# Pooled v with its keys on the partitions: by DMA through a scratch in HBM, or by copies and transposes

## The chip, the cores and the metric

The program runs on one core of a Trainium2 chip. The metric is the device time of one execution in microseconds, the median of several runs. TensorE (PE), VectorE (DVE), ScalarE (ACT), GpSimd (POOL) and SyncE (SP) each run their own instruction list in order and wait for each other on semaphores. SP computes nothing here: it issues nearly all DMAs, which all go into one queue that 16 DMA engines serve.

## What is computed

Three layers in a row, all in fp32:

```python
# attention, B=8 batches, H=8 heads, S=576 queries, D=64; keys and values pooled by 8 -> SP=72
k_p = k.reshape(B, H, Sp, 8, D).mean(axis=3);  v_p = v.reshape(B, H, Sp, 8, D).mean(axis=3)
attn = softmax(q @ k_p.T / sqrt(D))
x = (attn @ v_p)                       # as [4608, 512]
# soft mixture of experts: 32 slots, 8 experts, w1 [8,512,1024], w2 [8,1024,512]
logits = x @ phi
d = softmax(logits, over tokens);  slot_input = d.T @ x
slot_out[e] = relu(slot_input[e] @ w1[e]) @ w2[e]
x = softmax(logits, over slots) @ slot_out
# last layer: h = x @ w_in, h * softmax(h), layer norm, @ w_out
```

The kernel never builds `x`. For the logits it multiplies attn with (v_p @ phi). For the slot inputs it forms `dat = d.T @ attn` for each batch (32 slots by 72 keys of each head) and then `dat @ v_p`. The second product contracts over the 72 keys, so it needs v_p with its keys on the partitions: the tile `v72` [72, 8 heads, 64].

## The kernel before

**Stage 1, attention (about 0 to 178 us).** Loop over 8 batches `b`, each with 5 tiles of queries. The instruction lists of PE, ACT and DVE are written by hand as `step(b, par, t, ...)` with t = 1 to 5, software-pipelined: step t does the scores of tile t+2, the transposed q of tile t+3, the transposed attn of tile t and the logits of tile t-1. `par` is the parity of the batch and picks one of two buffers. Batch 0 is unrolled, batches 1 to 6 run in a loop of two batches a turn, and the last batch has a tail of its own.

**Loads.** For each batch SP loads v (two DMAs, `load_v`, lines 403 and 406), q (four `qb` DMAs of 1024 pieces of 256 bytes, line 427, and two `ql`, line 430), from batch 3 on also one 2 MB half of an expert's weights (`load_w`, lines 436 and 438), and k (two DMAs). The loop of SP is at lines 468 to 479: it waits until v of batch b is pooled (`v_pooled`), loads v and q of batch b+1 and a weight half, waits until k of batch b+1 is pooled and loads k of batch b+2. `load_v(7)` is in its iteration b=6. After it come the weight halves whose place in SBUF comes free late: n=5, n=7, n=6, then the output weights `wo_raw` (`load_out`, line 449: chunks 0 to 3, 4, 5 and 6, 7), parts of halves 8 (`wnine`) and 9 (`wten`), and, in stage 2, halves 10 to 15.

**Pooling.** `fold` (lines 380 to 394) adds the 8 neighbours in three levels; level 2 writes `kp` or `vp` and signals `k_pooled` or `v_pooled`. Most of it is done by POOL, between the normalisations of attn (`norm`, line 577).

**The way of v.** `vT_t` transposes `vp` on PE into the bank `b_head` (line 1419); `vT_evac` on ACT copies it into `vpad` (v transposed, with its pooled keys in the free dimension, 6 copies); `wphi_t` and `vphi_t` make v_p @ phi of it. For `v72`, the heads' columns are copied out of `vpad` into `vT`: `vT_close` on ACT for batches 0 and 1, `vT_copy` on DVE for the others (two copies of 64x288). Then `v72_t(b)` at step 2 transposes them back on PE (4 transposes, line 1459, behind three waits), and `v72_evac(b)` at step 3 copies the bank to `v72` on ACT. `slot_t(b)` reads `v72` at step 5 of the next batch (line 1553) and signals `slot_ps`.

**The tail of the last batch.** After step 1 of batch 7 PE goes through scores, logits and `dat_t` of batch 6, `lmax_t`, `slot_t(6)`, then waits for `wo_in0` (chunks 0 to 4 of `wo_raw`), runs `mb_t`, `col_sum(0)`, waits for `wo_in1` (chunks 5 to 7), runs `col_sum(1)` (line 1640, 8 matmuls each), `dat_t(7)`, `datT_t(7)` and `slot_t(7)`. The order is fixed, so everything after waits with it.

**Stage 2, experts (178 to 222 us):** `hid_t(e)` (line 1698) and `so_t(e)` (line 1720) for the 8 experts, each waiting for its half of the weights. **Stage 3 (from 222 us):** the last layer, 36 output tiles of 128 tokens, PE busy nearly throughout.

Of the kernel before, what the change touches and what calls it, by code (L numbers as in the profile page):

```python
# [29 lines left out]
F32 = mybir.dt.float32  # L30
# [5 lines left out]
P = 128  # L36
# [45 lines left out]
def build(nc, q, k, v, phi, w1, w2, w_in, w_out, g_ln, out):  # L82
    with ExitStack() as ctx:
# [40 lines left out]
        vp = bump("vp", [P, EVEN, D])  # L124
# [15 lines left out]
        vT = bump("vT", [P, PAIRS, SP])  # L140
        vT_end = place[0]
# [32 lines left out]
        assert attn_end + HALF // MC <= vpad_end and attn_end + 2 * HALF // MC <= vT_end  # L174
# [205 lines left out]
        def fold(engine, name, raw, pooled, b, level):  # L380
# [19 lines left out]
        def _(sp):  # L400
# [49 lines left out]

            load_first_k()
# [9 lines left out]
            sp.wait_ge(sem("v_pooled"), 1)  # L461
            load_v(1)
# [24 lines left out]
            load_w(3, 0)  # L487
            sp.wait_ge(sem("qT_ps"), B * TILES - 1)
# [3 lines left out]
            sp.wait_ge(sem("vT_closed"), B)  # L492
# [5 lines left out]
            sp.wait_ge(sem("v72_ps"), B)  # L498
# [55 lines left out]
        def _(pool):  # L554
# [14 lines left out]
            def v_fold(b, level):  # L569
                fold(pool, "v", vraw, vp, b, level)  # L570
# [9 lines left out]
            v_fold(0, 0)  # L580
# [5 lines left out]
            v_fold(1, 0)  # L586
            norm((0, 0, 3))

            def step(b, par, t, k_next, v_next):
                norm(ahead(b, par, t + 1))  # L590
                if t == 1 and v_next:
                    v_fold(b + 1, 1)
                    v_fold(b + 1, 2)
# [5 lines left out]
                if t == 5 and k_next:  # L599
                    v_fold(b + 2, 0)  # L600
# [82 lines left out]
        def _(act):  # L683
# [25 lines left out]
            def vT_close(b):  # L709

                act.wait_ge(sem("vT_sb"), b + 1)
                for hh in range(2):
                    c = 1 + hh * HEAD
                    last = copy(vT[hh * D:(hh + 1) * D, :, :], vpad[hh * D:(hh + 1) * D, :, c:c + SP])
                last.then_inc(sem("vT_closed"), 1)

# [30 lines left out]

            def v72_evac(b, par):
                act.wait_ge(sem("v72_ps"), b + 1)
# [1150 lines left out]
```

## Time and profile before

| | us |
|---|---|
| median of 3 runs (lowest, highest) | 452.81 (450.83, 453.76) |
| the profiled execution, first to last instruction | 449.2 |
| of it attention | about 178 |
| of it experts | about 44 |
| of it last layer | about 227 |

The granted TensorE clock is 1.00 of full speed in every stretch. PE is busy 96% of the span, VectorE 71%, ScalarE 60%, GpSimd 56%. The 16 DMA engines are busy for nearly the whole first 212 us. Durations of single instructions are pipelined: the busy time of a group of matmuls overlaps that of the next, so what a group adds to the time is read from the chain of work that ended last, where pieces don't overlap.

### The profile page before, as it was taken

What the parts mean: (1) busy time and instruction counts of PE and PEld (TensorE: products, weight loads), DVE (VectorE), ACT (ScalarE), POOL (GpSimd) and SP (SyncE); (2) the same over time, 40 slices, a digit from 0 to 9 for tenths busy, and PEclk for the clock granted to TensorE, in tenths of its full rate; (3) what the DMA queues carried; (4) which work ended last, traced back from release to release, by engine and by line L of the source; (5) the groups of instructions that cost most, each with busy time, mean ns of one, the idle gap of its engine ahead of it and who ended that gap; (6) DMA issues with size and microseconds to landing.
All of it is one profiled execution on the core that took longest, in us unless ns stands there. A gap on an engine that the chain in (4) does not pass through costs nothing.

```text
span 449.2 us, 10103 instructions
## 1 busy us (share of the span) xinstructions
PE 431.4 (96%) x3492; PEld 335.0 (75%) x3492; DVE 316.9 (71%) x558; ACT 267.4 (60%) x604; POOL 251.0 (56%) x347
## 2 busy tenths in 40 slices
PE   6899999999999998999899999999999999999997
PEld 6676787778778775445578788888888888888886
DVE  5888697877879665736598987777777777777311
ACT  2588878778787854134387665655565555666310
POOL 2569977878887230112034336766766667666540
PEclk9999999999999999999999999999999999999999
DMA  8969959898999998999500276676666766666642
GB/s 258 296 190 239 257 151 267 329 283 279 341 211 359 388 393 285 392 389 396 207 1 24 48 163 118 132 144 137 134 136 140 141 134 134 132 118 136 154 81 47
DMA packets 125951, 91.71 MB, mean 204 GB/s; under 512 B 105176, under 2 KB 105440, under 8 KB 124000
## 3 DMA queue, kind: packets, MB, share of 16 engines
q1 hardware_dynamic: 120752, 82.08, 66.8%
q10 hardware_dynamic: 5168, 9.24, 6.0%
q8 instruction: 17, 0.28, 0.3%
q14 instruction: 14, 0.11, 0.1%
HBM read 66.13 MB, written 9.44 MB: 168 GB/s over the span
## 4 chain that ended last, share of the span: by engine, by line
PE 75%; DVE 7%; ACT 6%; DMA 6%; issue 3%; POOL 1%; SPq 1%; DVEq 0%; ACTq 0%
PE banks L1835 13%; PE banks L1837 13%; PE banks L1836 13%; PE banks L1412 5%; DMA wslot<-in_moe_w 5%; PE banks L1475 3%; PE banks L1393 3%; PE banks L1807 3%; ACT vpad L685 2%; PE banks L1499 2%; PE banks L1535 2%; PE banks L1698 2%; PE banks L1506 2%; PE banks L1720 2%; DVE attn L1039 1%
## 5 line engine op out<-in xcount | busy, mean ns | idle before, releaser
L1835 PE MATMUL banks<-wo_hi,uh 128*128 128x512 f32 x280 | 109.6, 391 | 0.1
L1837 PE MATMUL banks<-wo_hi,ul 128*128 128x512 f32 x280 | 109.0, 389 | 0.0
L1836 PE MATMUL banks<-wo_lo,uh 128*128 128x512 f32 x280 | 108.9, 389 | 0.0
L653 POOL TENSOR_TENSOR ul<-u_col,uh 128x1024 fp32r<-128x1024 f32 x30 | 72.2, 2407 | 16.2 <-ACT uh L685 15.0
L577 POOL TENSOR_TENSOR attn<-attn,srec 128x576 f32<-128x576 f32 (+1 forms) x40 | 43.2, 1082 | 39.6 <-DVE srec L1051 39.4
L950 ACT ACTIVATE sq<-u,st 128x1024 f32<-128x1024 f32 x36 | 41.5, 1153 | 39.9 <-DVE u L1284 39.9
L1835 PEld LDWEIGHTS banks<-wo_hi,uh 128*128 128x128 f32 x280 | 52.6, 188 | 11.4 <-DVE ul L1301 0.5
L1837 PEld LDWEIGHTS banks<-wo_hi,ul 128*128 128x128 f32 x280 | 52.5, 188 | 11.0
L1836 PEld LDWEIGHTS banks<-wo_lo,uh 128*128 128x128 f32 x280 | 52.6, 188 | 10.7
L1284 DVE SCALAR_TENSOR_TENSOR u<-banks,ex 128x1024 f32<-128x1024 f32 x35 | 42.7, 1223 | 22.3 <-ACT ex L941 22.2
L1274 DVE TENSOR_REDUCE st<-banks 128x1 f32<-128x1024 f32 x35 | 42.6, 1218 | 17.5 <-PE banks L1807 17.5
L941 ACT ACTIVATE ex<-banks,st 128x1024 f32<-128x1024 f32 x35 | 39.0, 1114 | 17.1 <-DVE st L1274 16.7
L685 ACT ACTIVATE uh<-u_col 128x1024 fp32r<-128x1024 f32 x30 | 31.8, 1060 | 28.4 <-DMA u_col<-u_blk 14.5
L1315 DVE TENSOR_SCALAR osb<-banks,rs 128x512 f32<-128x512 f32 x35 | 26.0, 742 | 19.2 <-PE banks L1837 19.2
L1412 PE MATMUL banks<-kblk,qT 128*128 128x144 f32 x256 | 37.8, 291 | 1.0 <-DVE attn L1039 0.9
L1294 DVE STREAM_TRANSPOSE u_blk<-u 128x1024 f32<-128x1024 f32 x30 | 37.4, 1246 | 1.9
L1412 PEld LDWEIGHTS banks<-kblk,qT 128*128 128x128 f32 x256 | 33.1, 190 | 3.7 <-issue 3.5
L639 POOL TENSOR_SCALAR st<-st 128x1 f32<-128x1 f32 x36 | 6.9, 190 | 51.6 <-ACT sq L950 51.3
L1033 DVE TENSOR_REDUCE smax<-banks 128x8 f32<-128x576 f32 (+1 forms) x40 | 27.4, 685 | 10.9 <-PE banks L1412 10.5
L728 ACT ACTIVATE attn<-attn 128x576 f32<-128x576 f32 (+1 forms) x40 | 25.5, 636 | 14.8 <-DVE attn L1039 14.4
L1046 DVE TENSOR_REDUCE ssum<-attn 128x8 f32<-128x584 f32 (+1 forms) x40 | 27.8, 694 | 4.9 <-ACT attn L728 4.6
L685 ACT ACTIVATE aT<-banks 128x512 f32<-128x512 f32 (+1 forms) x80 | 28.7, 403 | 2.1 <-PE banks L1475 1.0
(197 smaller groups left out, 792.8 us busy)
## 6 DMA issues: line engine op xcount, KB each, us to landing
wslot<-in_moe_w SPq DMA_DIRECT2D x13, 2048.0 KB, 13.6
u_col<-u_blk SPq DMA_DIRECT2D x240, 64.0 KB, 2.2
qb<-in_q SPq DMA_DIRECT2D x32, 256.0 KB, 6.3
out<-osb ACTq DMA_DIRECT2D x32, 256.0 KB, 2.5
vraw<-in_v SPq DMA_DIRECT2D x8, 640.0 KB, 5.4
kraw<-in_k SPq DMA_DIRECT2D x7, 640.0 KB, 5.9
vraw<-in_v SPq DMA_DIRECT2D x8, 512.0 KB, 4.0
kraw<-in_k SPq DMA_DIRECT2D x7, 512.0 KB, 5.0
```

Of the source, the lines that this page charges most:

```text
L577: pool.tensor_tensor(a, a, per_head(srec[bit(tile)], t)[:, :, :, None].to_broadcast([P, tile_pairs(t), 2, SP]), ALU.mult) \
L653: pool.tensor_tensor(ul[par][:, :, :].rearrange("p c (q t) -> p (c q) t", q=4), v, uh[par][:, :, :].bitcast(F32).rearrange("p c (q t) -> p ...
L685: return act.activation(o, i, ACT.Copy, scale=scale)
L941: act.activation(ex[par][:, :, :], h_banks(par), ACT.Exp, bias=st[k % STATS]["nmax"][:, :], accum_out=st[k % STATS]["den"][:, :]).then_inc ...
L950: act.activation(sq[par][:, :], u[k % URING][:, :], ACT.Square, scale=-float(FF), bias=st[k % STATS]["usum"][:, :], accum_out=st[k % STATS ...
L1274: dve.tensor_reduce(st[k % STATS]["nmax"][:, :], h_banks(k % 2), AX.XY, ALU.max, negate=True).then_inc(sem("nmax"), 1)
L1284: dve.scalar_tensor_tensor(u[k % URING][:, :].rearrange("p (a n) -> p a n", a=2), h_banks(par), 1.0, ex[par][:, :, :], ALU.mult, ALU.mult, ...
L1294: dve.transpose(u_blk[slot][:, :, :, k % 2, :].rearrange("p c q t -> p (c q) t"), u[k % URING][:, :].rearrange("p (b f) -> p b f", f=BLK)) \
L1412: last = pe.matmul(s_view[:, j, 0:2 * SP], qT[bit(tile)][:, j, :], kblk[par][:, j, :], start=True, stop=True)
L1835: pe.matmul(ps[4 + par], uh[par][:, c, :], wo_hi[:, c, :], start=(c == 0), stop=False)
L1836: pe.matmul(ps[4 + par], uh[par][:, c, :], wo_lo[:, c, :], start=False, stop=False)
L1837: last = pe.matmul(ps[4 + par], ul[par][:, c, :], wo_hi[:, c, :], start=False, stop=(c == FC - 1))
```

## The change

`v72` no longer goes through `vT` and PE. As soon as `vp` is pooled, SP writes it to a scratch `pooled_v` in HBM (`spill_v`, two DMAs), and reads it back with the keys on the partitions (`load_v72`, five DMAs of 16 or 8 partitions). `vp` has two buffers. `vT`, `vT_close`, `vT_copy`, `v72_t` and `v72_evac` are gone. The division by 8 that `vT` carried moves to the accumulated denominator, at the end of the stage.

```diff
@@ tiles and the fold
-        vp = bump("vp", [P, EVEN, D])
+        vp = [bump("vp0", [P, EVEN, D])]
-        vT = bump("vT", [P, PAIRS, SP])
+        vp.append(bump("vp1", [P, EVEN, D]))
+                if name == "v" and not (isinstance(b, int) and b < 2):
+                    engine.wait_ge(sem("pooled_v_out"), (b - 1) * 32)
@@ SP
+            def spill_v(b):
+                for a, n in enumerate((EVEN, ODD)):
+                    sp.dma_start(row(pooled_v, b % 2)[0:n, :, a, :].rearrange("n i d -> i n d"), vp[b % 2][a::2, 0:n, :]).then_inc(sem("pooled_v_out"), 16)
+            def load_v72(b):
+                if b >= 2:
+                    sp.wait_ge(sem("slot_ps"), b - 1)
+                sp.wait_ge(sem("pooled_v_out"), 32 * (b + 1))
+                for n in range(EVEN):
+                    i = row(pooled_v, b % 2)[n].rearrange("(h g) a d -> (g a) h d", h=H)
+                    if n < ODD:
+                        c = 4 * POOL * (n % 2) + 2 * POOL * (n // 2)
+                        o = v72[b % 2][c:c + 2 * POOL, :, :]
+                    else:
+                        o, i = v72[b % 2][8 * POOL:SP, :, :], i[0::2]
+                    sp.dma_start(o, i).then_inc(sem(f"v72_in{b % 2}"), 16)
             sp.wait_ge(sem("v_pooled"), 1)
+            spill_v(0)
             load_v(1)
             load_q(1, 1, (1, 2, 3, 4))
             sp.wait_ge(sem("k_pooled"), 2)
             load_k(2)
+            load_v72(0)
             for b in range(1, 7):
                 sp.wait_ge(sem("v_pooled"), b + 1)
+                spill_v(b)
                 load_v(b + 1)
...
                     load_k(b + 2)
+                load_v72(b)
             load_w(2, 1)
+            sp.wait_ge(sem("v_pooled"), B)
+            spill_v(B - 1)
...
             load_w(3, 0)
+            load_v72(B - 1)
             sp.wait_ge(sem("qT_ps"), B * TILES - 1)
             load_out(0, WO_EARLY - 1, 0)
...
-            sp.wait_ge(sem("vT_closed"), B)
             load_part(8, 0, 1)
...
-            sp.wait_ge(sem("v72_ps"), B)
             load_part(8, 1, 2)
@@ ACT: v72_evac (step 3), vT_close (batches 0 and 1) removed
@@ DVE: vT_copy (step 4) removed
-            dve.tensor_scalar(accd1[:, :], acc_den[:, :], TINY, None, ALU.add)
+            dve.tensor_scalar(accd1[:, :], acc_den[:, :], TINY, float(POOL), ALU.add, ALU.mult)
@@ PE
-            def vT_t(b, early=False):
+            def vT_t(b, par):
                 pe.wait_ge(sem("v_pooled"), b + 1)
-                if early:
-                    pe.wait_ge(sem("kT_sb"), b + 1)
-                else:
-                    pe.wait_ge(sem("v72_sb"), b)
-                rows_T("vT", vp)
+                pe.wait_ge(sem("kT_sb"), b + 1)
+                rows_T("vT", vp[par])
-                if t == 2:
-                    v72_t(b)
@@ slot_t
-                pe.wait_ge(sem("v72_sb"), b + 1)
+                pe.wait_ge(sem(f"v72_in{par}"), (b - par) * 40 + 80)
@@ tail
-            v72_t(B - 1)
...
-            pe.wait_ge(sem("v72_sb"), B)
+            pe.wait_ge(sem("vphi_sb"), B)
```

In `pooled_v` (2, 5, 64, 2, 64) the row of 64 floats is the innermost dimension, and neighbouring rows belong to the two values of `a`, so each piece of a spill and of a load is 256 bytes: 576 pieces (147 KB) each way and batch.

## Rows read from the trace of the kernel before

**Rows 1.** Page, 40 slices of the span: busy tenths of PE and of the DMA engines
```profile
PE   6899999999999998999899999999999999999997
DMA  8969959898999998999500276676666766666642
```
**Rows 2.** Window of one batch: PE, PEld, DVE, ACT, POOL busy, clock, DMA, GB/s
```profile
84.70:104.15 19.45, 19.31 (x238) 15.16 (x238) 15.82 (x37) 15.50 (x49) 15.73 (x12) 1.00 0.98 290
```
**Rows 3.** Chain that ended last, in order of time (start, us): v72_t(1) and v72_t(6)
```profile
46.99 0.44 PE banks L1459 x4
...
145.25 0.44 PE banks L1459 x4
145.69 0.44 PE banks L1393 x4
```
**Rows 4.** Timeline (start, us): v72_t(7) and what follows; one batch's copies
```profile
164.32 0.61 PE L1459 MATMUL banks<-ident,vT 128*72 128x128 f32 x4
165.08 0.63 PE L1499 MATMUL banks<-aT,vphi 128*32 128x128 f32 x10 [0.15 <-ACT aT L685]
...
88.92 0.58 ACT L685 ACTIVATE v<-banks 72x512 f32<-72x512 f32 x1
...
95.12 0.96 DVE L1065 COPY vT<-vpad 64x288 f32<-64x288 f32 x2
```
**Rows 5.** Timeline of SP, iteration b=4 and the start of the next
```profile
85.41 0.47 SPq L403 DMA_DIRECT2D vraw<-in_v  x1
...
96.17 0.77 SPq L406 DMA_DIRECT2D kraw<-in_k  x1
104.85 0.47 SPq L403 DMA_DIRECT2D vraw<-in_v  x1
```
**Rows 6.** DMA packets: only q pieces, 111 to 114 us; then queue 1, 300 to 400 us
```profile
DMA packets 2608, 0.66 MB, mean 220 GB/s; under 512 B 2608, under 2 KB 2608, under 8 KB 2608
...
q1 hardware_dynamic: 36761, 8.86, 53.5%
```
**Rows 7.** GB/s in 40 slices of 1 us, from 112 us; then from 150 us
```profile
GB/s 217 219 215 259 410 397 406 414 455 430 420 51 0 57 147 391 389 304 273 217 218 218 196 142 328 336 383 354 371 414 422 426 414 403 393 389 383 385 387 387
...
GB/s 387 387 393 385 383 385 399 410 401 414 410 410 379 389 399 412 373 375 207 393 402 387 352 356 373 80 270 256 121 215 383 266 404 410 426 414 414 414 401 418
```
**Rows 8.** DMAs issued 75 to 77 us: KB, us to landing; and when POOL reads the k
```profile
kraw<-in_k SPq DMA_DIRECT2D x1, 640.0 KB, 10.7
...
88.29 2.92 POOL L386 TENSOR_TENSOR kraw<-kraw 128x1280 f32<-128x1280 f32 x1
```
**Rows 9.** Chain, in order of time: slot_t(4) and slot_t(5)
```profile
136.31 0.36 PE banks L1553 x16
...
155.74 0.36 PE banks L1553 x16
```
**Rows 10.** Timeline of SP, from v(7) to the last chunks of wo
```profile
124.69 0.47 SPq L403 DMA_DIRECT2D vraw<-in_v  x1
...
134.54 9.61 SPq L438 DMA_DIRECT2D wslot<-in_moe_w  x2
...
154.78 0.37 SPq L449 DMA_DIRECT2D wo_raw<-in_moe_w_out  x1
...
165.02 0.33 SPq L446 DMA_DIRECT2D wnine<-in_moe_w  x1
167.10 0.89 SPq L449 DMA_DIRECT2D wo_raw<-in_moe_w_out  x2
```
**Rows 11.** DMAs issued 167.4 to 169.2 us: KB, us to landing (the last chunk of wo)
```profile
wo_raw<-in_moe_w_out SPq DMA_DIRECT2D x1, 256.0 KB, 4.8
```
**Rows 12.** Timeline of PE: col_sum, dat_t(7) (PEld: weight loads of the second half)
```profile
172.48 1.92 PE L1640 MATMUL banks<-wo_raw,gT 128*32 128x512 f32 x16
...
173.37 0.13 PEld L1640 LDWEIGHTS banks<-wo_raw,gT 128*32 128x32 f32 x4 [0.30 <-issue]
...
216.20 1.92 PE L1720 MATMUL banks<-wslot,hz 128*32 128x512 f32 x16 [1.01 <-DMA wslot<-in_moe_w]
```

More of the change, by code:

```diff
@@ L79, with build @@
 FC = FF // P
-def build(nc, q, k, v, phi, w1, w2, w_in, w_out, g_ln, out):
+def build(nc, q, k, v, phi, w1, w2, w_in, w_out, g_ln, pooled_v, out):
     with ExitStack() as ctx:
@@ L139, in build @@
         vphi = [bump("vphi0", [P, NB, SLOTS])]
-        vT = bump("vT", [P, PAIRS, SP])
-        vT_end = place[0]
+        vp.append(bump("vp1", [P, EVEN, D]))
+        vp_end = place[0]
         vphi.append(bump("vphi1", [P, NB, SLOTS]))
@@ L567, in k_fold, with v_fold @@
                 fold(pool, "k", kraw, kp, b, level)
-            def v_fold(b, level):
-                fold(pool, "v", vraw, vp, b, level)
+            def v_fold(b, par, level):
+                fold(pool, "v", vraw, vp[par], b, level)
             def norm(tile):
@@ L746, in aT_evac @@
                 copy(o, i).then_inc(sem("aT_sb"), 1)
-            def v72_evac(b, par):
-                act.wait_ge(sem("v72_ps"), b + 1)
-                copy(v72[par][:, :, :], b_head[0:SP, :].rearrange("p (h d) -> p h d", d=D)).then_inc(sem("v72_sb"), 1)
             def alpha_exp(b, par):
@@ L805, in step @@
                     dat_evac(b - 1)
-                if t == 3:
-                    v72_evac(b, par)
                 if t == (2 if first else 1) and not last:
@@ L854, in _ @@
             dat_evac(B - 2)
-            v72_evac(B - 1, 1)
             datT_evac(B - 2, ps[0])
@@ L1058, in logit_evac @@
                 dve.tensor_copy(batch_logits(tile[0])[:, tile[2], :], l_bank(tile)[:, P:P + SLOTS]).then_inc(sem("l_sb"), 1)
-            def vT_copy(b):
-                dve.wait_ge(sem("vT_sb"), b + 1)
-                for hh in range(2):
-                    c = 1 + hh * HEAD
-                    last = dve.tensor_copy(vT[hh * D:(hh + 1) * D, :, :], vpad[hh * D:(hh + 1) * D, :, c:c + SP])
-                last.then_inc(sem("vT_closed"), 1)
             def vphi_evac(b, par):
@@ L1114, in _ @@
             sub_max((0, 0, 1))
-            fold(dve, "v", vraw, vp, 0, 1)
-            fold(dve, "v", vraw, vp, 0, 2)
+            fold(dve, "v", vraw, vp[0], 0, 1)
+            fold(dve, "v", vraw, vp[0], 0, 2)
             sub_max((0, 0, 2))
@@ L1145, in step @@
                     lmax_tokens(b)
-                if t == 4 and not first and not last:
-                    vT_copy(b + 1)
             c_rows = c_all[:, :, :, :].rearrange("p b t s -> p (b t) s")
@@ L1170, in _ @@
             dve.wait_ge(sem("den_acc"), B)
-            dve.tensor_scalar(accd1[:, :], acc_den[:, :], TINY, None, ALU.add).then_inc(sem("acc_rec"), 1)
+            dve.tensor_scalar(accd1[:, :], acc_den[:, :], TINY, float(POOL), ALU.add, ALU.mult).then_inc(sem("acc_rec"), 1)
             dve.wait_ge(sem("acc_rec"), 1)
@@ L1450, in vphi_t @@
                 pe.transpose(b_head[0:BLOCKS[4], 32 + 3 * P:96 + 3 * P], wphi[0:64, 4 * P:4 * P + BLOCKS[4]], ident[0:64, 0:64]).then_inc(sem("vphi_ps"), 1)
-            def v72_t(b):
-                pe.wait_ge(sem("vphi_sb"), b + 1)
-                pe.wait_ge(sem("vT_closed"), b + 1)
-                if not (isinstance(b, int) and b == B - 1):
-                    pe.wait_ge(sem("kT_sb"), b + 2)
-                for j in range(PAIRS):
-                    last = pe.transpose(b_head[0:SP, j * P:(j + 1) * P], vT[:, j, :], ident[:, :])
-                last.then_inc(sem("v72_ps"), 1)
             def aT_t(tile):
@@ L1575, in _ @@
             scores((0, 0, 2))
-            vT_t(0, True)
+            vT_t(0, 0)
             aT_t((0, 0, 0))
@@ L1598, in step @@
                 if t == 4 and first:
-                    vT_t(b + 1)
+                    vT_t(b + 1, 1 - par)
                 if not first:
@@ L1629, in step @@
                 if t == 3 and not last and not first:
-                    vT_t(b + 1)
+                    vT_t(b + 1, 1 - par)
                 if t == 4 and not last and not first:
```

29 lines of the change are left out of this document (10 added, 19 removed).

## The prediction

> **What bounds the kernel now.** I read the page first. Of its 40 slices the first 20 show two things busy together: PE, and the 16 DMA engines; after slice 20 the DMA engines have room and PE is the bound to the end [rows 1]. The change touches only the first part, so the question is which of the two sets the pace there.
>
> The window of one batch (84.70 to 104.15 us) says PE: 19.31 of 19.45 us busy, against 15 to 16 us for VectorE, ScalarE and GpSimd, at full granted clock [rows 2]. But in the same window the DMA engines are at 0.98. They keep up because every load is asked for about a batch ahead. The slices of 1 us show their reserve: in the batch that ends with the load of v(7), the queue runs empty from 123.1 to about 125.9 us, 2.8 us idle [rows 7]. From then on they are full until 175 us but for a dip at 168. Less work on PE is worth something only while loads stay ahead; the tail, where weights, wo and the last batch share the queue, is where I look for the end of that.
>
> **What is removed.** v72_t is 4 transposes. The group is shown as 0.61 us, but it overlaps its neighbours; on the chain that ended last it takes 0.44 us, and the next qT_t follows it without a gap (145.25 + 0.44 = 145.69) [rows 3]. There are six such pieces on the chain, for batches 1 to 6 (46.99, 66.44, 86.55, 105.98, 125.82 and 145.25 us). v72_t(0), at 27.96 us, is not on it: there the chain is POOL's fold of v(1) and DVE behind it. v72_t(7) is covered as well: the next group waits for ScalarE's aT anyway, until 165.08 us [rows 4]. So PE gets 6 x 0.44 = 2.64 us.
>
> The copies: v72_evac (0.58 us of ACT for each batch) and vT_copy (0.96 us of DVE, or 0.88 us of ACT in batches 0 and 1) [rows 4]. Both engines have 3.5 to 4 us of idle in a batch [rows 2], and PE stands still only 0.14 us in it. vT_copy holds back the sum behind it by about 0.4 us, which POOL's norm sees but PE doesn't, since that tile's transposes come a step later. I take nothing for them; 0.14 us a batch is all that PE could gain, under 1 us in all. If the cover goes (DVE on the path at that place), it is 0.4 us x 6 = 2.4 us, kept for a rival.
>
> The waits: v72_t's three and the one of vT_t on v72_sb had long been met in the steady batches. load_part(8,1,2) loses the wait that held it to 165.02 us [rows 10]; it goes out some 6 us earlier, and since the queue is full then, it only fills the dip at 168 (207 instead of about 390 KB in that us [rows 7], 0.5 us). The ALU.mult on accd1 rides on an instruction that exists: nothing.
>
> **What is added on SP.** Seven issues a batch. One costs 0.5 to 0.8 us [rows 5], so about 4.2 us. SP is done with a batch at 96.94 and idles to 104.85, 7.9 us [rows 5]: hidden, but for order. spill_v stands ahead of load_v, so v, q, weights and k are issued 1.2 us later. load_v72 stands last in the iteration and waits for slot_ps; what is queued behind it is only the next wait for v_pooled, later by 7 us. Two places differ. load_v72(6) waits for slot_t(4), 136.31 us [rows 9], and behind it is the weight half issued at 134.54 [rows 10]; load_v72(7) waits for slot_t(5), 155.74 us, and behind it are wo chunks that went out at 154.78. With 3 us of issues both come some 5 us late. At both places the queue holds 10 us and more of earlier halves (the load of wo at 154.78 was not served before about 162), so no engine runs dry: nothing.
>
> **What is added on the DMA engines.** 576 pieces of 256 bytes out and 576 in. No such write to HBM is in this trace. The nearest rows: q pieces, HBM to SBUF, moved at 220 GB/s while nothing else ran [rows 6], that is 18.6 ns a piece on each of 16 engines, 36 pieces each: 0.67 us. The five loads are 16 or 8 partitions wide; if the narrow one uses 8 engines, these have 40 pieces: 0.74 us. The SBUF to SBUF shuffle of stage 3: 36761 pieces took 53.5% of 100 us x 16 engines, 23.3 ns each [rows 6]: 0.84 us. I take 0.67 for a spill and 0.74 for a load, as the q pieces are the same size with the same memory, and bound both, below, by 0.37 (147 KB at the 400 GB/s of long pieces [rows 7], which no 256-byte piece here reaches) and, above, by twice the dearer row, 1.7 us, since HBM writes of this size are not shown.
>
> The Trainium skill (DMA: Bandwidth & Descriptors, Specifications) speaks against the change here: transfers under 512 bytes are below line rate, because the engine then reads, modifies and writes. For reading, the rows agree: 220 GB/s for 256-byte pieces beside about 390 for the weights' long ones. For a write to HBM no row of before shows it; read as a doubling of the spill, the sum below would come out 1.3 us later.
>
> In the steady batches the sum, 1.4 us, fits in the 2.8 us of reserve, less the 0.44 us by which the batch shrinks. k lands later by SP's 1.2 us: k of 75.53 us landed 10.7 later, at 86.2, and POOL read it at 88.29 [rows 8], so 2.1 us of slack covers it.
>
> **The tail, where it is decided.** The queue is full from v(7) to the last chunk of wo. So the landing of that chunk is a sum: it was issued at about 167.6 (the second of the pair at 167.10 [rows 10]) and landed 4.8 later [rows 11], at 172.4. It moves by:
> - the start of the full stretch. v(7) waits for v_pooled, behind v72_t(1) to (4): 4 x 0.44 = 1.76 us earlier;
> - spill(6) ahead of v(7): two issues, 1.2 us later (more than its 0.67 of data);
> - load(6), spill(7) and load(7) in the queue: 0.74 + 0.67 + 0.74 = 2.15 us later;
> - the dip at 168 filled: 0.5 us earlier.
>
> Sum: +1.1 us, 173.5 us. PE began the second half of col_sum, which needs this chunk, at 173.37 us [rows 12]. Without the transposes it would be there at 170.7, and wait. So PE's 2.64 us is lost in a wait of 2.8 us for wo, and the whole ends 0.1 us later: 449.2 + 0.1 = 449.3 us of span. Behind it dat_t(7), stage 2 and its last weights (gated by hid and so, on PE) move along; the last half was awaited 1.01 us at 216.20 [rows 12], and its issue depends on PE's progress too, so that stays. Against the median of 452.81, which is 3.6 above the profiled execution's span, the forecast is 453.0 us.
>
> **Rivals.**
> 1. *The wait for wo doesn't bite; PE keeps its gain.* For it: the wait is a difference of large sums, and 1 us of unseen reserve in the queue gives 1 us back (with all pieces at the lower bound of 0.37, wo lands at 172.4 and the end is 1 us earlier). Against: wo would have to land by 170.8, 1.6 us earlier than before, with 3 us more in front of it. 452.8 - 2.6 = 450.2 us.
> 2. *Small pieces are dearer, moderately.* If spills alone cost 1.7 us: the two tail spills add 0.5 + 1.0 us, wo lands at 175.0, the end is 1.6 us later, 454.4. If loads cost 1.7 too: another 1.9 us and about 1 us of backlog from before 125.9, end +4.5, 457.3.
> 3. *The DMA engines become the bound of the steady batches (the side of slower).* Once a spill and a load together exceed about 2.4 us (2.8 of reserve less 0.44), each batch with a weight half leaves a backlog, and once k comes over 2.1 us late POOL, then PE, wait. With a spill of 3.4 us (four times the shuffle's row) and a load of 0.74: 1.7 us of backlog in each of 3 batches, 5 us, and 6.8 + 1.5 - 2.3 = 6 us in the tail: wo at 183, some 9.5 us later, 462 us. It decides from a pair of 2.4 us on. For it: the DMA share of 0.98 [rows 2] and that the write is unseen. Against: neither 256-byte row is over 0.84 us.
> 4. *The freed DVE and ACT time was on the path.* 2.64 + 2.4 = 5.0 us faster, 447.8, and only if wo is in time. Against it: 0.14 us of idle PE in a batch.
>
> That slot_t waits for v72 instead, I exclude: the load goes out a batch and more ahead in the steady state, and in the tail about 20 us ahead of slot_t(7).
>
> **How the numbers follow.** A measurement of this kernel can tell about 1% (4.5 us) from no change. Forecast, within 1 us or so of before: 0.44. Rival 1: 0.16. Rival 2: 0.14. Rival 3: 0.16. Rival 4: 0.10. Within 1% are the forecast, rival 1 and rival 2: 0.74; slower is rival 3, 0.16; faster is rival 4, 0.10. The range takes in rival 1 at the low end (450.2, with the runs' own scatter 449.5) and most of rival 2 at the high end (456.5), which leaves out 0.26 less the near edges of rivals 3 and 4, about 0.2.
>
> **What would show it.** In the steady batches the chain goes from l_t straight to qT_t, and batches are 0.44 us shorter. The queue's idle stretch before v(7) shrinks from 2.8 to about 1 us. The landing of the spills and loads gives the price of a piece. In the tail PE stands 2 to 3 us before line L1640's counterpart, waiting for wo. Wrong would be: no wait there (rival 1), batches longer than before with POOL waiting for kraw (rival 3), or batches shorter by more than 0.6 us (rival 4).

## The result: 0.8% slower, and where the profile after shows it

| | before | after |
|---|---|---|
| median of the runs side by side, us | 451.84 (7 runs) | 455.9 (7 runs, 454.08 to 456.74) |
| ratio after / before | | 1.0079, 95% interval 1.0057 to 1.0102 |
| the profiled execution, us | 449.2 | 454.6 |
| mean granted TensorE clock of it | 1.000 | 0.988 |

The forecast was 453.0 us in a range of 449.5 to 456.5. The kernel after is 4.1 us slower than before by the medians, and 5.4 us by the two profiled executions. All of the 5.4 us, and the loss of what PE had gained before, arise between 168 and 184 us of the span.

First the timeline of PE after: start and duration in us, the line, and at the end of a row for how long the engine stood and what it waited for. The first two rows are `slot_t(0)` and `slot_t(5)`, the counterpart of L1553 in [rows 9]; the others are the tail, the counterpart of [rows 12].

```profile
57.15 0.43 PE L1536 MATMUL banks<-v,datT 72*32 72x64 f32 x16
...
152.69 0.43 PE L1536 MATMUL banks<-v,datT 72*32 72x64 f32 x16
...
168.29 0.43 PE L1536 MATMUL banks<-v,datT 72*32 72x64 f32 x16
173.66 0.60 PE L1504 MATMUL banks<-ident,slot_max 32*128 32x32 f32 x2 [4.93 <-DMA wo_raw<-in_moe_w_out]
174.19 1.94 PE L1621 MATMUL banks<-wo_raw,gT 128*32 128x512 f32 x8
176.93 1.93 PE L1621 MATMUL banks<-wo_raw,gT 128*32 128x512 f32 x8 [0.81 <-DMA wo_raw<-in_moe_w_out]
178.64 2.42 PE L1518 MATMUL banks<-attn,dexp 128*32 128x147 f32 x40
...
184.02 1.93 PE L1678 MATMUL banks<-wslot,slotT 128*32 128x256 f32 x32
```

**The steady batches** are shorter. From `slot_t(0)` to `slot_t(5)` are 95.54 us, 19.11 a batch. Before, the same way took 98.26, 19.65 a batch. So a batch is 0.54 us shorter, where [rows 3] promised 0.44. The two rows of before:

```profile
57.41 0.43 PE L1553 MATMUL banks<-v,datT 72*32 72x64 f32 x16
...
155.67 0.43 PE L1553 MATMUL banks<-v,datT 72*32 72x64 f32 x16
```

`slot_t(6)` is at 168.29 and not 171.28: PE comes to the tail 3.0 us earlier.

**The tail** takes it back twice over. PE stands 4.93 + 0.81 = 5.7 us for `wo_raw`. The chain that ended last (start, us, what) has the same from the other side. Its first three rows are the place of the removed transposes, where `qT_t` (L1389) now follows at once; the others say that the last chunk of wo, issued at about 165.5 us, landed 11.4 us later, at 176.9 (before: at 172.4, [rows 10, 11]).

```profile
122.60 0.70 PE banks L1458 x5
123.30 0.32 PE banks L1489 x2
123.62 0.47 PE banks L1389 x4
...
165.51 11.38 DMA wo_raw<-in_moe_w_out
...
176.93 1.93 PE banks L1621 x8
178.87 2.19 PE banks L1518 x40
```

And the work behind the wait is slower: 8 matmuls of `col_sum` take 1.93 us, where before 16 took 1.92 [rows 12], and the 40 of `dat_t(7)` take 2.42, where before they took 1.43. The windows show why (columns: window, length, busy time of PE, PEld, DVE, ACT and POOL, granted clock, DMA share, GB/s):

```profile
168.00:170.00 2.00, 0.65 (x24) 0.52 (x24) 0.50 (x3) 0.05 (x1) 0.00 (x0) 1.00 1.04 344
170.00:172.00 2.00, 0.00 (x0) 0.00 (x0) 0.00 (x0) 0.00 (x0) 0.00 (x0) 0.60 1.04 402
172.00:174.00 2.00, 0.34 (x2) 0.37 (x2) 0.00 (x0) 0.00 (x0) 0.00 (x0) 0.50 1.03 397
...
178.00:180.00 2.00, 2.00 (x30) 1.11 (x24) 0.00 (x0) 0.00 (x0) 0.00 (x0) 0.50 0.62 248
180.00:182.00 2.00, 2.00 (x32) 1.49 (x25) 0.47 (x3) 0.30 (x2) 0.00 (x0) 0.84 0.31 113
```

While PE stood, the granted clock went from 1.00 to 0.50, the 1.2 GHz level in place of 2.4, and it was still there when the work came. The sum of the tail: the second half of `col_sum` starts at 176.93 and not 173.37 (+3.56), takes 0.86 us more until `dat_t(7)` starts (1.71 and not 0.85), and `dat_t(7)` takes 0.98 more until the next group starts (2.35 and not 1.37). 3.56 + 0.86 + 0.98 = 5.4 us; `hid_t(0)` (L1678) starts at 184.02 and not 178.61, +5.4.

What the DMA engines did, in GB/s: 40 slices of 1 us from 112 us, then from 150 us, as in [rows 7].

```profile
GB/s 274 220 142 215 217 192 154 410 389 381 406 430 451 416 306 201 364 420 374 266 230 215 206 221 99 344 317 365 391 338 428 420 410 434 401 355 207 201 351 391
...
GB/s 351 391 391 383 348 386 409 403 393 379 416 406 406 410 418 339 171 253 291 397 399 406 401 393 387 387 401 412 385 111 25 201 332 170 244 387 381 363 324 369
```

The idle stretch before v(7) (before: 51, 0, 57 GB/s at 123 to 125 us) is gone. There are two dips in the full stretch, at 147 to 150 us and at 165 to 168. Both are loads. The DMA packets under 512 bytes show whose pieces moved when; first from 146 to 150 us, then from 154 to 156:

```profile
DMA packets 972, 1.16 MB, mean 291 GB/s; under 512 B 649, under 2 KB 649, under 8 KB 972
...
DMA packets 888, 0.73 MB, mean 367 GB/s; under 512 B 599, under 2 KB 599, under 8 KB 888
```

The first 649 belong to load(6), issued from 136.29 us on, and the 599 after them to spill(7), issued from 142.26 us on. Experiments 5 and 6 confirm it: with spills alone there are 608 small packets at 152 to 154 us and hardly a dip (365 GB/s over the two), and with loads alone there are the dips, in each case with the small packets in them. Load(6) is priced so: 355, 207, 201 and 351 in place of 390 are 0.45 MB short, 1.1 us, and its own 147 KB would have taken 0.4 more: 1.5 us. Load(7), with 339, 171, 253 and 291, gives 1.3 + 0.4 = 1.7 us. Spill(7), with 348 and 386, is 0.05 MB short: 0.1 + 0.4 = 0.5 us, little more than its bytes.

Last, GpSimd and SP. Timeline of POOL, the counterpart of the second line of [rows 8]; there are four such waits, 10.0 us together, where before had none. That sum is of one execution: experiments 3, 4 and 8, whose steady batches run the same instructions, have 4.8, 6.3 and 4.8 us of them (from 50 us on). Two of the four:

```profile
90.39 2.90 POOL L386 TENSOR_TENSOR kraw<-kraw 128x1280 f32<-128x1280 f32 x1 [3.23 <-DMA kraw<-in_k]
...
110.16 2.90 POOL L386 TENSOR_TENSOR kraw<-kraw 128x1280 f32<-128x1280 f32 x1 [3.96 <-DMA kraw<-in_k]
```

Timeline of SP, from v(7) to the last chunks of wo, the counterpart of [rows 10]:

```profile
124.16 1.31 SPq L456 DMA_DIRECT2D pooled_v<-vp  x2
125.52 0.67 SPq L405 DMA_DIRECT2D vraw<-in_v  x1
...
136.29 4.49 SPq L470 DMA_DIRECT2D v<-pooled_v  x5
...
142.26 7.70 SPq L456 DMA_DIRECT2D pooled_v<-vp  x2
...
156.84 2.13 SPq L470 DMA_DIRECT2D v<-pooled_v  x5
159.02 0.54 SPq L451 DMA_DIRECT2D wo_raw<-in_moe_w_out  x1
...
165.02 2.57 SPq L451 DMA_DIRECT2D wo_raw<-in_moe_w_out  x2
```

v(7) is issued at 125.52 and not 124.69, and the two issues of the last spill take SP 7.70 us, where those of the one before took 1.31.

### The profile page after: what moved, and what is told of

It reads as the page before. It is cut to its first block, busy times and chain, and to the rows that moved or that the text cites. A ratio compares the mean times of both kernels' runs of the same rounds, so it can differ in the third digit from the quotient of the medians.

```text
span 454.6 us, 10070 instructions
## 1 busy us (share of the span) xinstructions
PE 432.0 (95%) x3460; PEld 332.7 (73%) x3460; DVE 310.7 (68%) x546; ACT 262.5 (58%) x592; POOL 251.0 (55%) x347
## 4 chain that ended last, share of the span: by engine, by line
PE 67%; DMA 8%; DVE 8%; ACT 5%; issue 5%; POOL 4%; SPq 2%; DVEq 0%; POOLq 0%
PE banks L1815 12%; PE banks L1816 12%; PE banks L1817 12%; DMA wslot<-in_moe_w 4%; PE banks L1408 4%; PE banks L1458 3%; PE banks L1787 3%; PE banks L1389 3%; DMA wo_raw<-in_moe_w_out 3%; PE banks L1518 2%; PE banks L1678 2%; SPq L560 2%; PE banks L1482 2%; ACT vpad L710 2%; PE banks L1489 2%
## 5 line engine op out<-in xcount | busy, mean ns | idle before, releaser
L1816 PEld LDWEIGHTS banks<-wo_lo,uh 128*128 128x128 f32 x280 | 52.6, 188 | 10.7
L641 POOL COPY cs<-c_all 128x640 f32<-128x640 f32 x8 | 5.7, 722 | 45.8 <-DVE c_all L1194 26.7
```

The lines of the kernel that those rows point to most:

```text
L1816: pe.matmul(ps[4 + par], uh[par][:, c, :], wo_lo[:, c, :], start=False, stop=False)
```

## The experiments

All ratios are to the kernel before on the same chip, with 95% intervals. "Theory A" and the rest are named in the expectations themselves. Each diff is against the kernel after unless it says otherwise.

The profiled executions differ already before the steady batches: `slot_t(0)` starts at 57.15 us in the kernel after and up to 1.7 us later in others. So the places late in the span are best counted from `slot_t(0)` of the same execution. In us, read from the timelines and the DMA issues:

| kernel | `slot_t(0)` at | to v(7) issued | to last chunk of wo landed | to `hid_t(0)` |
|---|---|---|---|---|
| before | 57.41 | 67.3 | 115.0 | 121.2 |
| after | 57.15 | 68.4 | 119.8 | 126.9 |
| no traffic (1) | 58.88 | 65.3 | 112.6 | 118.5 |
| clock held (4) | 58.42 | 66.7 | 119.9 | 125.2 |
| spills alone (5) | 58.54 | 66.8 | 115.8 | 121.1 |
| loads alone (6) | 58.66 | 65.3 | 115.9 | 122.9 |
| wo first (8) | 58.09 | 66.7 | 113.6 | 120.0 |

**1. The removals alone.** From batch 2 on nothing is spilled or loaded; `slot_t` then reads stale values, so this kernel leaves the way of v out. The waits that belong to the removed DMAs are changed with them.

```diff
-                spill_v(b)
+                if b < 2:
+                    spill_v(b)
-                load_v72(b)
+                if b < 2:
+                    load_v72(b)
-            spill_v(B - 1)
-            load_v72(B - 1)
```

> The changed kernel without its traffic: spills and loads of the scratch only for batches 0 and 1, so the later batches use stale values of v in the slot inputs. It keeps what the change takes away (transposes, copies). Theory A (the traffic delays the last chunks of wo, PE's gain is real but lost there): PE reaches the tail some 3 us early and wo is in time or nearly; 2 to 3 us faster than the kernel before. Theory B (the removed work was covered anyway and the tail is set by something else): within 1 us of the kernel before. A would also show POOL without waits for kraw.

Measured: 449.18 us, ratio 0.9946 (0.9921 to 0.9972): 2.4 us faster than before. In its timeline of PE, `col_sum` is one group at full clock and waits for nothing:

```profile
171.21 1.92 PE L1619 MATMUL banks<-wo_raw,gT 128*32 128x512 f32 x16
172.95 1.43 PE L1516 MATMUL banks<-attn,dexp 128*32 128x147 f32 x40
```

Its profiled execution, 449.1 us, is no shorter than before's, because it reached `slot_t(0)` 1.5 us later; from there to `hid_t(0)` it is 2.7 us shorter. GpSimd has no wait for kraw in the steady batches. So the removals are worth about what the prediction said (2.64; the interval of the ratio is 1.3 to 3.6 us), and all the rest, 1.33% or about 6 us between this kernel and the one after, is the traffic and its issues. How much less the queue carries is in the DMA packets from 140 to 165 us, a stretch in which it is full; first the kernel of this experiment, then the one after:

```profile
DMA packets 3836, 9.94 MB, mean 398 GB/s; under 512 B 96, under 2 KB 96, under 8 KB 3835
```

```profile
DMA packets 4838, 9.47 MB, mean 379 GB/s; under 512 B 1320, under 2 KB 1320, under 8 KB 4837
```

The kernel after moves 0.47 MB less in the 25 us, and 0.29 MB of what it moves are the pieces of load(6) and spill(7): 0.76 MB of other data is missing, at 398 GB/s 1.9 us for the two. The dips gave 1.5 and 0.5. The same packets with spills alone are 9.89 MB, 0.5 us for one spill; with loads alone they are 9.05 MB, 3.0 us for two loads.

**2. PE's work put back.** Four transposes of the identity at the places of `v72_t`.

```diff
+            def same_work(b):
+                ...
+                for j in range(PAIRS):
+                    pe.transpose(b_head[0:SP, j * P:(j + 1) * P], ident[:, 0:SP], ident[:, :])
...
                 l_t(before)
+                if t == 2:
+                    same_work(b)
```

> The changed kernel with four transposes of the identity at each place where v72_t stood (the same PE time, 0.44 us a batch; their output isn't used), all traffic kept. Theory A: DMA sets the landing of wo, so PE's wait for it shrinks by what the transposes take (4.9 us to about 2.5) and the end stays within 1 us of the changed kernel. Theory B (PE sets the pace after all): 2.6 us slower than the changed kernel, 6.5 slower than before.

Measured: 456.41 us, ratio 1.0095 (1.006 to 1.013), 0.5 us over the kernel after, within the intervals. The work went into the wait, which shrank from 4.93 to 2.23 us (PE came to it 3.7 us later, 1.7 of that from the start of the execution and 2.0 from the transposes, and wo landed 1.0 later):

```profile
174.65 0.60 PE L1511 MATMUL banks<-ident,slot_max 32*128 32x32 f32 x2 [2.23 <-DMA wo_raw<-in_moe_w_out]
177.93 1.93 PE L1630 MATMUL banks<-wo_raw,gT 128*32 128x512 f32 x8 [0.81 <-DMA wo_raw<-in_moe_w_out]
```

What sets the end of stage 1 in the kernel after is the landing of wo, not PE. This is the core of the prediction, and it holds. The run also splits the shorter batch: from `slot_t(0)` to `slot_t(5)` it takes 97.57 us, so five batches lose 2.03 us by the transposes (0.41 each) and 0.69 (0.14 each) by what else is gone.

**3. The last load behind wo.**

```diff
-            load_v72(B - 1)
+            sp.wait_ge(sem("pooled_v_out"), 32 * B)
...
             load_out(FC - 1, FC, 1)
+            load_v72(B - 1)
```

> The changed kernel with load_v72(7) moved behind the last chunk of wo in SP's order; nothing else. Theory A: wo has five DMAs less ahead of it and lands earlier by their price, 0.7 us (by the q pieces) to 1.5 us (by the rates in the trace of the change); the end comes 0.7 to 1.5 us earlier than that of the changed kernel. Theory C (the lateness is all made in the steady batches, by SP's late issues and k): no change.

Measured: 455.65 us, ratio 1.0097 (1.0064 to 1.013): no gain that can be told. Its profiled execution waits for wo 2.18 and 2.51 us, 4.7 in all and not 5.7. One load less in front of wo is worth about 1 us in the trace and disappears in the scatter of the times. The move took little out of the way: the small pieces of this load went through the queue from 171 to 175 us, and the last chunk of wo landed only at 175.6.

**4. The clock held.** 40 and 16 identity transposes of no use ahead of the two waits for wo, so that PE is busy while it waits.

```diff
             slot_t(B - 2, 0, ps[0][:, 256:512])
+            keep_clock(b_aT[0], 40)
             pe.wait_ge(sem("vphi_sb"), B)
...
             col_sum(0)
+            keep_clock(b_aT[0], 16)
             pe.wait_ge(sem("wo_in1"), 32)
```

> The changed kernel with 40 transposes of the identity ahead of PE's wait for wo_in0 and 16 ahead of that for wo_in1 (0.11 us each, in time that PE waits anyway). In the changed kernel the granted clock was 0.5 from the wait to 180.65 us, and col_sum and dat_t took twice their time, 1.0 + 1.0 + 0.9 us more. Theory A with a clock term: the clock stays at 1.0, the part behind the landing is about 1.9 us shorter, 1.5 to 2 us faster than the changed kernel. Without it (the landing alone decides): no change, or slower where the filler is longer than the wait.

Measured: 454.65 us, ratio 1.0071 (1.0045 to 1.0097). The granted clock was 1.0 in four of its five executions and 0.996 in one; the kernel after had 0.988 to 0.992 in all seven. `dat_t(7)` is back at 1.43 us:

```profile
178.31 1.06 PE L1621 MATMUL banks<-wo_raw,gT 128*32 128x512 f32 x8 [0.52 <-DMA wo_raw<-in_moe_w_out]
179.19 1.43 PE L1518 MATMUL banks<-attn,dexp 128*32 128x147 f32 x40
```

The groups in the trace differ by 1.9 us, and from `slot_t(0)` to `hid_t(0)` this execution takes 1.7 us less. The two medians differ by 1.3 us, the ratios to before by only 0.4, and their intervals overlap. So the trace shows the clock's share, and the times only don't contradict it.

**5 and 6. Spills alone, loads alone.** From batch 2 on only the one half of the traffic (and stale values in `v72`).

```diff
# spills alone
-                load_v72(b)
+                if b < 2:
+                    load_v72(b)
-            load_v72(B - 1)
# loads alone
-                spill_v(b)
+                if b < 2:
+                    spill_v(b)
-            spill_v(B - 1)
```

> The changed kernel with all spills, but loads of v72 only for batches 0 and 1 (the later batches use stale values of v). Without any traffic it took 449.2 us, with all of it 455.9. Theory W (the write of short pieces to HBM is the dear half): 453 to 455 us. Theory L (the loads into 16 partitions are the dear half): 450 to 451. Theory E (both alike, 1.2 to 1.6 us each): 451.5 to 453, and wo waited for 1 to 3 us.

> The changed kernel with all loads of v72, but spills only for batches 0 and 1 (the loads read stale values from the scratch). Theory W: 450 to 451 us. Theory L: 453 to 455. Theory E: 451.5 to 453.

Measured: spills alone 452.56 us, ratio 1.0030 (0.9998 to 1.0063); loads alone 453.0 us, 1.0022 (0.9997 to 1.0047). Against the kernel without traffic (0.9946) that is +0.84% and +0.76%, and both together +1.33%. By the times the halves cost about the same, 3.8 and 3.4 us when alone, each with an interval of some 2 us to either side. Together they cost 0.3% less than the sum of the two, which is within the intervals. A part of each is the clock: 8 of the 10 executions with spills alone and 9 of the 10 with loads alone were below 0.999, without traffic 4 of 10.

The traces show that they cost it in different places. Counted from `slot_t(0)`, wo lands 3.3 us later with loads alone than without traffic, and two loads at 1.6 us in the queue are all of it. With spills alone it lands 3.2 us later, but a spill takes only 0.5 us of the full queue. 1.4 us are there when v(7) is issued, behind the issues of spill(6); the rest was not followed. The forecast's fear that writes of 256 bytes would be much dearer than reads is turned round: in the queue the write is the cheap half. In the loads-alone profile each load shows, in GB/s from 136 us, as a dip, at 145 to 147 and at 162 to 165 us:

```profile
GB/s 309 395 375 387 424 418 422 401 405 247 194 252 387 383 391 385 389 389 379 391 385 395 422 414 389 410 362 202 213 326 383 418 383 406 391 387 381 410 403 403
```

247, 194 and 252 for 390 are 0.48 MB, 1.2 us, and 0.4 for its own bytes: 1.6 us a load.

**7. Longer pieces in the spills alone.** Experiment 5 with a scratch in which each of 64 partitions writes one piece of 1280 or 1024 bytes.

```diff
+                    if b < 2:
+                        o = row(pooled_v, b % 2)[0:n, :, a, :].rearrange("n i d -> i n d")
+                    else:
+                        o = row(long_v, b % 2)[a, :, 0:n, :]
+                    sp.dma_start(o, vp[b % 2][a::2, 0:n, :])...
```

> As the run with spills only, but from batch 2 on the spill goes to a scratch laid out by partition, so that each DMA moves 64 pieces of 1280 or 1024 bytes instead of 320 or 256 pieces of 256 bytes: the same bytes, the same two issues. If the shortness of the pieces makes the price of a spill, this takes 449.5 to 450.5 us, close to the run without traffic (449.2). If the issue on SP or the write to HBM as such does, it takes what the run with short spills takes.

Measured: 451.48 us, ratio 0.9995 (0.9963 to 1.0028), against 1.0030 with short pieces. The intervals overlap widely. The two issues of the last spill took 1.84 us and not 3.69. Taken for itself this is a hint of 1.5 us, no more. In the queue there is little for it to save: the long pieces pass at 150 to 153 us with no dip (387, 394 and 414 GB/s), 0.4 us for their bytes, and the short ones took 0.5. Experiment 9 tries it in the full kernel.

**8. wo first.** SP issues all chunks of wo ahead of the last load and of the two parts of weight half 8.

```diff
-            load_v72(B - 1)
+            sp.wait_ge(sem("pooled_v_out"), 32 * B)
             sp.wait_ge(sem("qT_ps"), B * TILES - 1)
             load_out(0, WO_EARLY - 1, 0)
-            ... load_part(8, 0, 1)
             ...
             load_out(FC - 1, FC, 1)
+            load_v72(B - 1)
+            ... load_part(8, 0, 1)
+            ... load_part(8, 1, 2)
```

> The changed kernel with all its traffic; only the order of SP's loads in the tail is another: all chunks of wo first, then load_v72(7), then the two parts of half 8 (1 MB, 2.6 us of the queue, needed at 193 us). Theory A (the end is set by the landing of wo's last chunk, which PE awaits): wo lands 3 to 4 us earlier, PE's wait shrinks from 5.7 to 1 or 2 us, the clock doesn't fall, 450 to 452 us. Rival (the loss is made in the steady batches, the wait in the tail only shows it): within 1 us of the changed kernel's 455.9.

Measured: 454.13 us, ratio 1.0032 (1.0005 to 1.0059); the kernel after had 1.0079. In the profiled execution wo landed some 6.2 us earlier, counted from `slot_t(0)`, and the wait for it is gone. A part of the time comes back in stage 2, at the last weights. Timeline of PE:

```profile
171.95 1.92 PE L1622 MATMUL banks<-wo_raw,gT 128*32 128x512 f32 x16
173.69 1.43 PE L1519 MATMUL banks<-attn,dexp 128*32 128x147 f32 x40
...
211.99 1.93 PE L1679 MATMUL banks<-wslot,slotT 128*32 128x256 f32 x32 [0.87 <-DMA wslot<-in_moe_w]
217.39 3.35 PE L1701 MATMUL banks<-wslot,hz 128*32 128x512 f32 x16 [1.67 <-DMA wslot<-in_moe_w]
```

The intervals of 1.0032 and 1.0079 just touch. `hid_t(0)` started at 178.08 us, 5.9 earlier than in the kernel after, but the last `so_t` (L1701) only 3.5 earlier, at 217.39, after waits of 0.87 and 1.67 us for the last halves of the weights, and at the lower clock, 3.35 us for 1.92. Of the two waits the 1.67 is not new: the kernel without traffic waits 1.65 us at the same place. New are the 0.87 and the clock, which fell after this wait and not in the kernel without traffic. Nor is the wait for wo gone for good: in this execution PE was itself late, because its clock had been at 0.50 from about 163.1 to 166.5 us, and the profiles of experiments 9 (with wo first) and 10 stand 2.7 and 3.2 us for wo again.

**9. Long pieces in the full kernel, and together with wo first.** The scratch is laid out as [partition, half, group, 64] with one edit; a spill writes 1280 or 1024 bytes a piece, a load still reads 256.

```diff
-                    sp.dma_start(row(pooled_v, b % 2)[0:n, :, a, :].rearrange("n i d -> i n d"), vp[b % 2][a::2, 0:n, :])...
+                    sp.dma_start(row(pooled_v, b % 2)[:, a, 0:n, :], vp[b % 2][a::2, 0:n, :])...
-                    i = row(pooled_v, b % 2)[n].rearrange("(h g) a d -> (g a) h d", h=H)
+                    i = row(pooled_v, b % 2)[:, :, n, :].rearrange("(h g) a d -> (g a) h d", h=H)
```

> The changed kernel with one edit: the scratch laid out so that a spill writes pieces of 1280 and 1024 bytes; the order of SP stays. Theory I (pieces of the spills cost 1 us on the way to wo): 454.6 us, ratio 1.004 to 1.005, and the issue of the last spill takes 2 to 4 us in place of 7.7. Theory J (bytes and loads alone): 455.9, ratio 1.008, as the changed kernel. A third: reading 256 byte pieces with strides of 2560 bytes costs the loads what the spills gain, also 1.008, with the load issues stretched beyond 2.1 to 4.5 us.

> The kernel with wo issued ahead of the last load (load_v72(7) and the two parts of weight 8 behind it), and the scratch laid out so that a spill writes pieces of 1280 and 1024 bytes (the loads still read pieces of 256 bytes). Theory I (what is left over the kernel before, 1.5 us, is DMA work: pieces of 256 bytes in the spills, worth 1 us as between the two spill-only kernels): 453.0 us, ratio 1.001, and the waits of TensorE for the last weights (L1701, 1.7 and 0.9 us with wo first alone) together about 1 us shorter. Theory J (what is left is the bytes and the loads' pieces, the spills' pieces were noise): 454.1, ratio 1.003, as without the new layout.

Measured: long pieces alone 456.03 us, ratio 1.0095 (1.0073 to 1.0117), no gain over the 1.0079 of short ones. With wo first 452.88 us, 1.0002 (0.9983 to 1.002), against 1.0032 with short ones; again the intervals overlap. In the trace with long pieces alone, GpSimd waits 4.5 us for k (10.0 before the edit), the last spill's issue takes 4.67 us (7.70), and the first wait for wo is 2.97 and not 4.93. The first two are no sign of the edit: with short pieces experiment 8 has 4.8 and 4.74 us. Timeline of PE:

```profile
172.15 0.60 PE L1504 MATMUL banks<-ident,slot_max 32*128 32x32 f32 x2 [2.97 <-DMA wo_raw<-in_moe_w_out]
175.42 1.93 PE L1621 MATMUL banks<-wo_raw,gT 128*32 128x512 f32 x8 [0.81 <-DMA wo_raw<-in_moe_w_out]
177.13 2.68 PE L1518 MATMUL banks<-attn,dexp 128*32 128x147 f32 x40
```

That is 2 us less wait in one profiled execution, in six timed ones there was none to see. Theory I is not confirmed for the kernel as it stands. With 0.5 us for a short spill and 0.4 for a long one in the full queue (experiments 5 and 7), nothing in the traces supports the 1 us. The loads cost the same as before, 1.5 and 1.6 us (255, 190 and 283 GB/s at 146 to 148 us; 222, 196, 277 and 369 at 164 to 167), so the third theory, that they lose by the strides of 2560 bytes, falls too.

**10. The spill behind v.** On top of wo first and long pieces:

```diff
                 sp.wait_ge(sem("v_pooled"), b + 1)
-                spill_v(b)
                 load_v(b + 1)
+                spill_v(b)
```

> The kernel with wo first and long pieces in the spills, and in the loop SP issues load_v(b+1) ahead of spill_v(b) in place of behind it. Theory K (the spills' 1.3 us of issue ahead of v make v, q and k late, GpSimd waits 4 us for each k, and that is what makes the start of the last weights late): waits of GpSimd for kraw fall from 4 us to under 3 each, v(7) is issued 1 us earlier, ratio 0.998 to 0.999. Rival (k's lateness is the queue's own work, not the order): waits for kraw as before, ratio as without the move (1.001).

Measured: 452.23 us, ratio 1.0002 (0.9982 to 1.0022), as without the move. v(7) went out at 123.17 and not 125.12 us, but 1.4 of these 1.95 us are the earlier start of the execution, and the waits for kraw were 8.4 us in all (7.4 without). Theory K falls: the spill's place in front of v is not what makes k late. SP's four q issues took as long as before the move (7.3 us in each of three batches, against 7.4, 7.0 and 6.4), which speaks for the rival, a fuller queue, but no run isolates it.

**11. And the clock held.** On top of that, 14 and 8 identity transposes before the waits for wo.

> The last kernel (wo first, long pieces in the spills, spill behind v) with identity transposes of no use to the result in front of the two waits for wo, 14 and 8, about 1.6 and 0.9 us at 0.11 us each, to keep TensorE busy where it stood 2.9 and 0.3 us. If the granted clock at 1.2 GHz is what a short stand at this place costs: granted clock of the profile 0.996 to 1.0, the x40 group that follows takes 1.4 us and not 2.3, median 450.8 to 451.5, ratio 0.997 to 0.999, the first version ahead of the kernel before. If the time that the clock gives back is lost again in the wait for the last weights (L1701, whose arrival DMA sets), the clock rises and the ratio stays 1.000, and that wait grows from 0.9 to some 2 us.

Measured: 451.9 us, ratio 0.9994 (0.9972 to 1.0015), granted clock 1.0 in the profile. Timeline of PE, the waits for wo and for the last weights:

```profile
174.46 1.06 PE L1622 MATMUL banks<-wo_raw,gT 128*32 128x512 f32 x8 [0.62 <-DMA wo_raw<-in_moe_w_out]
175.34 1.43 PE L1519 MATMUL banks<-attn,dexp 128*32 128x147 f32 x40
...
217.01 1.92 PE L1703 MATMUL banks<-wslot,hz 128*32 128x512 f32 x16 [0.72 <-DMA wslot<-in_moe_w]
```

The wait for the last weights did not grow (0.72 us), and the median is 0.3 us under the 452.2 of the run before it, which is nothing that can be told. This is the best version with the change in it: level with the kernel before, and 0.48%, some 2 us, over the kernel without traffic. No version here beats the kernel before.

## Why the prediction was right, and which terms were not

**The mechanism held.** The steps "PE gets 2.64 us" (2.4 measured as time in experiment 1), "steady batches get shorter", "the tail decides" and "PE's gain is lost in a wait for wo" are what the trace shows, and experiment 2 shows the last: PE's work put back costs 0.5 us or nothing. The verdict, no change within 1%, holds with 0.79%, but its interval reaches 1.02%. There is luck in it: the forecast was a shift of +0.1 us, and the shift is 4.1. The range was wide enough to hold it, and that the time was missed by only 2.9 is the lower median of before in the new runs. It missed because the landing of wo moved by 4.5 us, not 1.1, and because the clock was not in the sum.

**The price of a load** was the term taken too low: 0.74 us. The dips give 1.5 to 1.7, just inside the upper bound of 1.7 and more than double the price of the q pieces in [rows 6]. The spill, at 0.67, was taken too high: 0.5 us. In the tail the three in front of wo are 1.5 + 0.5 + 1.7 = 3.7 us and not 2.15, +1.55. For the loads the row was not the right one. It was taken where q pieces had the queue to themselves; here short pieces stand among long ones, and they come in five DMAs of 8 or 16 partitions. Which of the two makes them dear was not tried; the spills stand among long pieces too and are cheap, and the layout of the scratch made no difference (experiment 9). The Trainium skill (DMA: Bandwidth & Descriptors, Specifications) says that pieces under 512 bytes are below line rate because of a read-modify-write. The reads of 256 bytes are slow here too. The writes of 256 bytes to HBM took 0.5 us where their bytes at the long pieces' rate are 0.4, so the doubling that I drew from it for spills is not what happened.

**The start of the full stretch** was to come 0.56 us earlier (1.76 for the transposes, less 1.2 for the spill's issue). v(7) was issued 0.8 us later. In this profile the step that failed is "k lands later by SP's 1.2 us ... 2.1 us of slack covers it": k of iteration 3 was issued at 79.30 us, 3.8 later than before, because spill, v and the load of the batch before stand in front, and the q issues are held up by a full queue (the four `qb` of the next iteration took 7.79 us, where before 5.10). GpSimd then waited 3 to 4 us for each k, and `v_pooled`, which opens SP's next iteration, came late with it. Experiments 3, 4 and 8 issue v(7) 66.6 to 66.7 us after `slot_t(0)`, earlier than before's 67.3, with GpSimd waits of 4.8 to 6.3 us; so this lateness is not in every execution. The mechanism is that of rival 3, and it set in at a pair price of 2.0 to 2.2 us, below the 2.4 from which it should decide. It went only as far as v: PE did not slow down, its five batches took 95.54 us in the kernel after and 95.54 (58.88 to 154.42) without traffic, because the slack behind GpSimd was enough. So rival 3's consequence was too large by the chain behind POOL, which I had not followed to PE.

**The sum again, with the measured terms:** start +0.8 in place of -0.56 (+1.4), three pieces of traffic +1.55. 1.1 + 1.4 + 1.55 = 4.05 us, measured 4.5. It closes to half a us and no better. The issue of v(7) is an early mark of the start: the q pieces behind v end at 136.3 us and not 134.7, 1.6 later, and with this the sum is 4.9. And in experiment 4 wo lands as late as in the kernel after although v(7) is issued earlier, so what the start is worth stays open. PE's delay from wo follows as predicted: 4.5 less the 1.0 us that the chunk had lain there before PE used it, 3.5 us.

**The clock** was missing. The forecast had PE stand 2.8 us and continue at full clock. It stood 5.7 us, and the next 48 matmuls of the path ran at the 1.2 GHz level: about 1.9 us by their durations, which the times of experiment 4 can't tell from nothing. A forecast that puts a stall on PE has to add this term.

**Rivals.** Rival 2 (dearer pieces) had named 454.4 for spills and 457.3 for both at 1.7 us. Its half on the spills is wrong and its half on the loads right, and 455.9 lies between the two figures; it came nearest, together with the start of rival 3. Rival 1 and rival 4 did not occur: there is a wait, and the freed time of DVE and ACT bought 0.14 us in a batch (experiment 2), the whole of PE's idle time there that the prediction had named.

## What to carry to other kernels

Work that is moved from an engine to DMA is not free where the queue has 2 to 3 us of reserve in a batch: price each direction by what it takes from a full queue (here, for 147 KB in 576 pieces, about 1.6 us to read them back and 0.5 to write them, where long pieces would take 0.4 at 390 GB/s), and follow that to the last transfer that an engine waits for. Before a dip is given to a transfer, look at whose pieces moved in it. Order what is left so that the chunk with the nearest deadline goes out first; here that came out 0.47% better, with intervals that just touch, and then the last weights, 40 us later, were waited for. And count a stall of PE together with what it does to the clock for the work behind it.

## What the runs showed of the hardware that was not expected

- In the kernel after, PE's last work before the wait ended at 168.7 us; the granted clock was 1.00 until 170 and 0.50 from 172 on (2.4 to 1.2 GHz), and it stayed there to 180, while PE worked 2.00 of 2.00 us in the last of these windows. With identity transposes in the wait it stayed at 1.00. Shorter waits were followed by the lower level as well: after 1.6 and 1.1 us for wo (wo first with long pieces) the 40 matmuls of `dat_t(7)` took 2.17 us. But the length of the wait alone does not decide. With spills alone PE stood 0.90 and 1.91 us and stayed at 1.00. At the last weights the kernel without traffic waited 1.65 us and stayed at 1.00, and wo first waited 1.67 and fell to 0.50 (windows of the first, then two of the second):

```profile
216.00:218.00 2.00, 2.00 (x19) 0.64 (x12) 0.75 (x2) 0.00 (x0) 0.10 (x1) 1.00 0.88 346
...
216.00:218.00 2.00, 0.61 (x8) 0.22 (x12) 1.29 (x3) 1.26 (x3) 0.00 (x0) 0.94 1.05 414
218.00:220.00 2.00, 2.00 (x16) 0.36 (x8) 0.11 (x1) 0.00 (x0) 0.00 (x0) 0.50 0.68 268
```

- The mean clock of an execution comes in steps (about 1.0, 0.996, 0.992, 0.988, 0.985). The kernel before has the first two: its 8 runs at 0.995 or 0.996 had a median of 453.1 us, and its 9 runs at 0.999 or 1.0 one of 451.3 (beside experiment 11). The scatter of one kernel's times goes with this step.
- An issue on SP took 0.45 to 0.65 us on a queue with room and up to 4.3 us on a full one: two issues of a spill took 1.31 us at 124 us and 7.70 at 142 (4.7 to 6.5 in the other executions with all traffic). With 128 long pieces in place of 576 short ones they took 1.84 and not 3.69 us (spills alone).
- 640 KB of k landed 10.4 to 11.9 us after issue, nearly as before (10.7): its lateness came from its issue.
